# Attention, channel mix and gated convolution on one core: short warm-up products, an earlier first normalisation, and another half whose strided values come in two parts

## The reference

```
scores = q @ k.T / 8                  # per batch and head
mask_local   = (rel >= 0) & (rel < 32)                # heads 0 to 3
mask_strided = (rel >= 0) & (pos_k % 32 == pos_q % 32)  # heads 4 to 7
attn = softmax(scores where the mask holds);  x = attn @ v
...
xk = mu_k * x + (1 - mu_k) * x_prev;  xr = mu_r * x + (1 - mu_r) * x_prev
x2 = sigmoid(xr @ w_r) * (relu(xk @ w_k) ** 2 @ w_v)
...
h = relu(x2 @ w_in);  gate = sigmoid(conv over 3 positions of h)
out = (h * gate) @ w_out
```

## Time and profile before

| | |
|---|---|
| median of 3 runs | 529.71 us (527.69 to 530.45) |
| the profiled execution, its own time | 526.64 us |
| its span | 524.8 us |
| TensorE busy | 516.7 us of the span, 6202 products |
| VectorE busy | 322.5 us |
| ScalarE busy | 287.6 us |
| GpSimd busy | 114.7 us |

### The profile page before, as it was taken

The page is one execution under the profiler, slowest core; times in us unless marked ns, Lnnn a source line. Parts: engine busy times, 40 slices in busy tenths (PEclk is TensorE's granted clock), DMA queues, the critical chain, the costliest instruction groups (busy, mean ns, idle before and its releaser), DMA issues.

```text
span 524.8 us, 15350 instructions
## 1 busy us (share of the span) xinstructions
PE 516.7 (98%) x6202; PEld 479.0 (91%) x6202; DVE 322.5 (61%) x812; ACT 287.6 (55%) x783; POOL 114.7 (22%) x139
## 2 busy tenths in 40 slices
PE   8799999999999999999999999999999999999997
PEld 6578999999999999999999999988998899889985
DVE  5769986657657566657644736881497049707910
ACT  4389288296394592691880815751583057416720
POOL 8039973031021040140221791000000000000000
PEclk9999999999999999999999999999999999999999
DMA  9893424343243332341106136001301130010011
GB/s 191 205 278 54 73 79 68 63 94 65 57 96 65 90 62 52 83 69 41 49 2 252 45 90 208 2 0 61 110 1 34 48 110 0 36 45 0 0 40 60
DMA packets 98772, 39.07 MB, mean 74 GB/s; under 512 B 91156, under 2 KB 91284, under 8 KB 98708
## 3 DMA queue, kind: packets, MB, share of 16 engines
q1 hardware_dynamic: 94334, 33.16, 25.6%
q0 software_dynamic: 1632, 4.36, 2.5%
q10 hardware_dynamic: 2742, 0.66, 0.8%
HBM read 28.72 MB, written 9.44 MB: 73 GB/s over the span
## 4 chain that ended last, share of the span: by engine, by line
PE 92%; SPq 6%; DMA 1%; issue 0%; ACT 0%
PE ps L788 19%; PE ps L798 19%; PE ps L680 9%; PE ps L681 9%; PE ps L682 8%; PE ps L731 7%; PE ps L732 7%; PE ps L733 6%; SPq L338 3%; PE ps L556 2%; PE ps L618 2%; PE ps L666 2%; SPq L350 2%; PE ps L599 1%; DMA vl<-in_v_dram 1%; SPq L383 1%
## 5 line engine op out<-in xcount | busy, mean ns | idle before, releaser
L492 POOL TENSOR_TENSOR k_lo<-k,k_hi 128x288 fp32r<-128x288 f32 x64 | 59.4, 931 | 192.6 <-ACT k_hi L860 192.5
L1275 DVE SCALAR_TENSOR_TENSOR cbuf<-hbuf,cols_c,cbuf 128x576 f32<-128x576 f32 x64 | 52.4, 819 | 63.5 <-ACT cbuf L965 62.4
L731 PE MATMUL ps<-k_hi,wb_hi 128*128 128x288 f32 x256 | 76.2, 298 | 0.0
L732 PE MATMUL ps<-k_lo,wb_hi 128*128 128x288 f32 x256 | 75.6, 295 | 0.0
L733 PE MATMUL ps<-k_hi,wb_lo 128*128 128x288 f32 x256 | 75.5, 295 | 0.0
L680 PE MATMUL ps<-xk_hi,wa_hi 128*128 128x288 f32 x224 | 67.1, 300 | 0.0
L681 PE MATMUL ps<-xk_lo,wa_hi 128*128 128x288 f32 x224 | 66.2, 295 | 0.0
L682 PE MATMUL ps<-xk_hi,wa_lo 128*128 128x288 f32 x224 | 66.1, 295 | 0.0
L798 PE MATMUL ps<-wb_hi,g_hi 128*128 128x512 f32 x144 | 57.5, 399 | 0.0
L798 PE MATMUL ps<-wb_hi,g_lo 128*128 128x512 f32 x144 | 56.8, 394 | 0.0
L798 PE MATMUL ps<-wb_lo,g_hi 128*128 128x512 f32 x144 | 56.5, 392 | 0.0
(11 more groups left out here) (110 smaller groups left out, 1160.5 us busy)
## 6 DMA issues: line engine op xcount, KB each, us to landing
x2d<-x2s SPq DMA_DIRECT2D x8, 576.0 KB, 3.1
x2raw<-x2d SPq DMA_DIRECT2D x4, 1152.0 KB, 5.2
out_dram<-ob SPq DMA_DIRECT2D x16, 256.0 KB, 2.0
raw<-in_q_dram SPq DMA_DIRECT2D x96, 36.0 KB, 1.9
raw<-in_k_dram SPq DMA_DIRECT2D x96, 36.0 KB, 1.9
wk_raw<-in_moe_w_k_dram SPq DMA_DIRECT2D x4, 512.0 KB, 9.2
wv_raw<-in_moe_w_v_dram SPq DMA_DIRECT2D x4, 512.0 KB, 5.9
ws<-in_moe_w_in_dram POOLq DMA_DIRECT2D x4, 512.0 KB, 7.2
```

Of the source, the lines that this page charges most:

```text
L492: nc.gpsimd.tensor_tensor(k2_lo[:, m], k2[:, m % K2RING], k2_hi[:, m].bitcast(F32), ALU.subtract).then_inc(k2_done, 1)
L731: nc.tensor.matmul(dst, wb_hi[:, f, cols], k2_hi[:, f, :], start=(f == 0), stop=False)
L732: nc.tensor.matmul(dst, wb_hi[:, f, cols], k2_lo[:, f, :], start=False, stop=False)
L1275: nc.vector.scalar_tensor_tensor(out=c, in0=h[:, o:o + S], scalar=conv[:, o, m:m + 1], in1=c, op0=ALU.mult, op1=ALU.add).then_inc(conv_ste ...
```

## The change

The diff has three parts. In the opening, the six warm-up products of 512 columns ahead of the first values become 48 of 64 columns. VectorE normalises block (0,0) ahead of the maxima of block (0,2), copies its values out before it normalises block (0,1), and local values of half 0 wait only for the maxima of the two local blocks. The half whose strided values are split over slots 12 and 13 is half 3 and no longer half 7.

```diff
+    WARM_MORE, WARM_LESS = 48, 64
...
-                wait(pe, maxed, tiles_at(h + 1))
+                wait(pe, maxed, tiles_at(h + 1) if h or kind == STR else tiles_at(0, 2))
...
-                    if h == NH - 1 and blocks(h)[i][0] == STR:
+                    if h == 3 and blocks(h)[i][0] == STR:
                         values(h, i, 0)
...
-                    if h == NH - 1 and blocks(h)[i][0] == STR:
+                    if h == 3 and blocks(h)[i][0] == STR:
                         values(h, i, 1)
...
-            keep_warm(WARM_SLOT + WARM_SLOT // 2)
+            keep_warm(WARM_MORE, WARM_LESS)
             values(0, 0)
             values(0, 1)
...
-                    if not (h == NH - 1 and blocks(h)[i][0] == STR):
+                    if not (h == 3 and blocks(h)[i][0] == STR):
                         copy_out(h, i)
...
-                    if h == NH - 1 and blocks(h)[i][0] == STR:
+                    if h == 3 and blocks(h)[i][0] == STR:
                         copy_out(h, i)
...
             mask_and_max(0, 1)
+            normalize(0, 0)
             mask_and_max(0, 2)
-            normalize(0, 0)
+            copy_out(0, 0)
             normalize(0, 1)
-            copy_out(0, 0)
             copy_out(0, 1)
```

## The result

The changed kernel takes 536.02 us at the median of 4 runs (533.88 to 537.06), the kernel before 528.86 us (527.69 to 530.45, 4 runs). The ratio is 1.0135, with a 95% interval of 1.0109 to 1.0160: slower, by 7.2 us where 4.4 were forecast. The forecast time of 534.1 stood on a median before of 529.71 from three runs; the fourth brought it down to 528.86. The profiled execution took 535.87 us with a span of 534.0, against 526.64 and 524.8 before: 9.2 us more in either.

The account below looks back on a forecast made before the run. TensorE, busy 516.7 of 524.8 us, was taken to bound the kernel, its opening held by late instruction blocks. A 4.4 us delay, other parts hidden or zero, added to the 529.71 median gave 534.1 us, range 530.2 to 537.

Parts of the forecast that it names:

- it now stands 84 instructions earlier: Opening: the instruction border from 22.03 us moves to four pairs before the end of values (0,1); block usable at 22.03.
- the sum's landmark: Opening: values (0,2) begin at 26.2 us instead of 21.61, 4.6 us later.
- the sum: Opening's late instruction block, with the small halt of 0.17 us gone: 4.4 us later in all.
- The likeliest case: Opening: delay as summed, TensorE's clock unhurt: 534.1 us, own range 533 to 535.5; chance 0.50.
- the second rival: Opening: delay as summed, and TensorE's clock falls to 1.2 GHz in the idle time: 535.6 us; chance 0.17.
- its signs: Opening: halts at 13.87 and four pairs before values (0,1) end; packet near 19.2 to 20.5; later distance to end unchanged.
- As TensorE waits for nothing afterwards, all of it reaches the end: Behind the start of values (0,2): the opening's 4.4 us delay passes whole into the kernel's end.
- The mechanism: TensorE's instruction stream: blocks of 256 instructions; on entering one block, the block after it is asked for.
- Sum zero: Strided values: two pieces cost 0.41 us, paid in half 3 and saved in half 7.
- about 0.1: Opening: without the missing block's cover, VectorE's chain up to `pt` of block (0,1) is about 0.1 us later.
- The price of a short product: Opening: 0.01 to 0.10 us for each of 43 short products, hidden behind the missing block, costing nothing.
- The rival by the Trainium skill: Opening: instruction blocks don't matter; time moves +0.1 to +2.3 us, 529.8 at the short end; chance 0.11.

Follow-up runs that it names:

- the padded kernel: Kernel before, opening untouched, with 42 products of 64 columns on zeros (84 instructions) added in the middle of half 0: 532.33 us, ratio 1.0091.

## Why the prediction was right in its direction and short by 3 us

**The border in the opening: right, to the instruction.** The step "it now stands 84 instructions earlier" put the halt four pairs before the end of values (0,1), and there it is. The block came at 20.68 and not at 22.03, and the sum's landmark, values (0,2) at 26.2, was met at 26.06. But it was met by luck, by two errors that cancel: without the fall of the clock the chain from 20.68 would have ended near 24.8 (the 1.35 us of the earlier block). The last four passes took 0.47 us instead of the 0.22 assumed and L667's group 3.24 instead of 2.18, which makes up for it; the warm-up products, 1.89 us instead of about 1.0, only fill the wait for VectorE. The likeliest case had the clock unhurt; what happened is the second rival, in each of the four profiled executions with 48 short products and the new order. Its price of 1.5 us was near the 1.3 measured, but its reason was weak: the rows of the warm-up products that it reads as half speed have 1.00 in their own clock column. In the three other of these executions the opening was late by another way. The first block came at 15.2 to 16.5 us and not at 13.9, the halt before the end of values (0,1) was 0.3 us or less, and values (0,2) began at 27.7 to 28.3. The prediction took the first block's time as fixed. Of its signs, the halts stood where it said, but the packet lay at 18.0 to 19.2 and not at 19.2 to 20.5, and the distance from values (0,2) to the end was not that of before.

**"As TensorE waits for nothing afterwards, all of it reaches the end": the step that failed.** The delay did reach the end, but the sentence took for granted that nothing new would appear behind the opening. The mechanism was applied to the borders of the opening and not to the some forty behind them. Half 1's strided values are 352 instructions in 1.9 us; in the kernel before only one border lies inside. In the changed kernel TensorE reaches one border at 53.08, inside the run, and the next stands behind pass 174, which costs 2.4 us, and up to 3 more at half clock. That is the 5.4 us that the sum lacked. Padding that leaves the opening untouched shows it alone: 2.4 us in its profile, and 3.5 at the median (4.7 less the 1.2 of its own products).

**"Sum zero" for halves 3 and 7: right by its result, wrong as a rule.** The 0.41 us were measured as forecast (half 3 plus 0.41, half 7 minus 0.41), but only because the borders had moved. With the old borders the same edit costs 4 us. I had priced the split by its own rows and not asked why it stood in half 7.

**VectorE's order at "about 0.1": mis-sized.** Alone it costs 1.7 us. The estimate took TensorE's values (0,0) as ready when VectorE wants to copy them; the first block of instructions comes between 13.5 and 16.8 us in the profiles, and with the copy ahead of the normalisation TensorE waits 1.82 to 1.85 us between the two local blocks in all seven profiles with the new order, whenever the block came. In the kernel before this wait was 0.26 us. In the changed kernel's first profile it is the wait at 17.57, hidden behind the missing block; in the three later ones, where that halt was 0.3 us or less, it was not hidden.

**The price of a short product**, 0.01 to 0.10 us: 43 took 1.43 us, 0.033 each, hidden as forecast in the first profile. In the three later ones they took 2.0 to 2.4 us, partly at half clock, and with hardly a halt behind them nothing hid that.

**The rival by the Trainium skill**, "Runtime: NRT & Kernel Launch", instruction fetch mechanics, that a border is "mostly hidden": over ordinary products it is in these traces, as in half 1 of the kernel before, where the border at 55.99 has no halt; with two borders in a run of short products it costs 2.1 us to 2.9.

**The total.** The short products alone make 8.5 us, the order alone 1.7, the split alone 4.0, together 14; the change loses 7 to 8. They don't add: the split in half 3 takes away the loss of 0.7 us that the short products alone cause there, half 7 no longer needs a split, and the new order hides in part behind the other losses of the opening. How much of the opening's loss belongs to each part was not measured. The profiled executions differ by 9.2 us where the medians differ by 7.2, because that before was 2.2 us faster than its median.

**What stays open.** Why the first block arrives anywhere between 13.5 and 16.8 us was not tried; the transfers of the opening are the same in all kernels. The opening's 4 to 8 us therefore mix a late first block, the short products, the order and the clock. Nor is it settled why the clock falls in some executions at a halt of about 2.3 us (half 1 of the changed kernel) and not in others (the profiled one of the padded kernel). When exactly a block is asked for is argued, not shown: in half 1 the packet begins 1.0 us behind the border at 53.08, but behind the border at 57.02 the next begins only at 61.09. No version beat the kernel before.

## What to carry to other kernels

An engine's instructions arrive in blocks, and a long run of very short instructions can consume one faster than the next comes. Count TensorE's instructions, with weight loads, passes and waits that stand by themselves, and ask of each row of short products whether two borders fall inside it; every instruction inserted ahead moves all borders behind it, so an edit at the start can cost time some forty microseconds later or in another half. Cut such a run in two with ordinary products between, and check again after each edit, because a kernel that runs without halts may owe it to its present count. And a wait with no engine as its cause inside a group that waits for nothing is the sign to look for.

## What the runs showed of the hardware that I had not expected

The halts that have no engine as cause and stand inside the local and strided values are exactly 256 instructions, or a multiple, apart from the first one (256 and 1536 in the changed kernel). A border in half 1 of the changed kernel that TensorE reaches at 53.08 us has its next block usable at 57.0, with the DMA engines at 0.23 of their capacity in the halt; in the opening it took 8.2 us in the kernel before and 7.2 in the changed one, with the engines at 0.92 and 0.96. The clock fell to half in halts of 1.7 to 3.8 us or up to 1.6 us behind them, and the work then ran at half speed for 3 to 10 us. In half 1 the halt cost its own length where the clock held (2.1 us, 2.4 lost) and more than twice that where it fell (2.4 us, 5.4 lost; with the short products alone 2.2 us, 5.3 lost).
